# First tile of a fused attention and expert kernel: weight pieces, copies and zeros moved

## The chip, the cores and the metric

The kernel runs on one core of a Trainium2 chip. The metric is device time in microseconds (us). Engines are called TensorE, VectorE, ScalarE, GpSimd and SyncE; in the profile's rows they are PE (PEld for its weight loads), DVE, ACT, POOL and SP.

## What is computed

Three layers run one after the other: attention that keeps the 32 largest scores of a row, a gated FFN behind an RMS norm, and a switch of 8 experts, each token going to one of them.

```python
# q, k, v: (2, 8, 576, 64)
scores = scale * q @ k.T
kth = np.partition(scores, -32, axis=-1)[..., -32:-31]
scores = np.where(scores >= kth, scores, -1e9)
attn = softmax(scores); x = attn @ v          # -> (1152, 512)

xn = x / rms(x) * rms_g
x = (silu(xn @ w_gate) * (xn @ w_val)) @ w_out # d_ff 1536

e = argmax(x @ r_gate); p = softmax prob of e  # 8 experts
y = relu(x @ w1[e]) @ w2[e]; out = p * y       # capacity 288 rows an expert
```

## The kernel before

Tokens are cut into 9 tiles of 128 (`NT`). A group `g` is one pair of heads of one tile: 4 groups a tile (`HP`), 36 in all (`NG`). All engines walk the same list of slots `n` (0 to `SLOTS` - 1), and each has its own instruction order in a slot, written out by hand; they meet in semaphores only.

The attention is a pipeline over the slots. VectorE in slot n finds the 32 largest of each score row of group n (`vec.max` and `vec.match_replace`, L1160 to L1181, on rows of 576, two heads of 128 rows each). In slot n + 1 GpSimd makes the clip bias and the negative row maximum from that (`nbias`, L1335 and L1339). ScalarE marks what lies below the threshold (`marks`, L919), GpSimd takes the marks off the scores (the clip, L1348), ScalarE takes the exponentials (`probs`, L929) and copies the next group's scores out of PSUM (`score_rows`). TensorE makes those scores (`scores`, L452), turns the probabilities (`turn_probs`, L463) and multiplies them with the values (`values`, L479) at the slot's end. `out_columns` copies that product to `oT`; it comes a slot later, behind the marks. The product shares a bank of PSUM with the scores, so `scores(n + 1)` waits for it (L446).

The FFN of tile t lies in the same slots. `due(n, at, k)` tells whether step k of some tile falls in slot n at the place ALPHA, BETA or GAMMA (start, middle, end); tile t counts from slot `FIRST` + 4t, and `FIRST` is 6. So for tile 0: step XA (-4) is slot 4, end. There the attention columns of three head pairs are turned back (`turn_back_columns`), copied (`raw_rows`), normalized on GpSimd (`norm_first`, L1305 to L1310) and turned again (`turn_first_rows`); ScalarE then scales them by the gain into `x_hi` (`columns`). Step XB (-3) is the start of slot 5: the last pair's columns are turned (L555), copied (`raw_last_pair`), normalized (`norm_last`), turned (L557) and scaled; `squares` (L893) sums the squares for the RMS, which GpSimd finishes (`rms`), and VectorE makes the low parts `x_lo` (`low_part`, L1109). The gate blocks are `G` (slots 5, 6, 7), the value blocks `V` (slots 6, 7, 7), each of 12 matmuls (L496, L497, L500); the tanh (L798), the SiLU product on VectorE (L1101) and the multiply on GpSimd (L1293) follow. Then the output product (L509), the router and the dispatch of the tile's rows by an indirect DMA.

TensorE multiplies in `float32r` with operands split in a high and a low part. The FFN's weights are split on the chip, in 12 pieces of 128 x 1024 (`split_piece`): pieces 0, 1 are the first column block of `w_gate`, 2, 3 that of `w_val`, 4, 5 and 6, 7 the second blocks, 8, 9 and 10, 11 the third. ScalarE rounds a piece to its high part in two copies (`split_weights`), and GpSimd subtracts that from the piece (L1285). Both happen at the place that `SPLITS` names for the piece. On GpSimd the piece stands in `dense`, behind the slot's clips and ahead of the next slot's bias. Block i of tile 0 waits for the low parts it needs (L489).

SyncE issues the loads in a fixed order: keys, queries, values of batch 0, keys of batch 1, the gain, `w_gate`, `w_val`, the router; then 18 stores of zeros to the dispatch buffer and 9 to the output (L342 to L346), from `zrow`, the first 520 columns of `hid`. ScalarE waits for these stores in `squares(0)`, since it writes `hid` there. Then `w_out`, the next queries and the values of batch 1. `drow` is the row buffer in which tiles 0 to 7 put their FFN output before the dispatch.

At the end the experts run one after the other from their dispatched rows (L707, L721).

Of the kernel before, what the change touches and what calls it, by code (L numbers as in the profile page):

```python
# [47 lines left out]
LAST = 16  # L48
SPLITS = ((2, ALPHA), (2, GAMMA), (3, BETA), (3, GAMMA), (4, ALPHA), (4, GAMMA),
          (5, BETA), (5, GAMMA), (6, ALPHA), (6, BETA), (6, GAMMA), (7, ALPHA))  # L50


def build(nc, q, k, v, w_gate, w_val, w_out, rms_g, r_gate, w1, w2, out, capacity):
# [31 lines left out]
    with ctx:  # L85
# [52 lines left out]

        zrow = hid[:, 0:ROW]

# [40 lines left out]
        def gate_of(e, j):  # L181
# [15 lines left out]

            "k_turned k_acted k_veced k1_copied w_hi_set w_lo_set "

# [65 lines left out]

        def pieces(n, at):

            m = SPLITS.index((n, at)) if (n, at) in SPLITS else None
            return () if m is None else (m,)

# [27 lines left out]
        def _(sp):  # L298
# [44 lines left out]
            for i in range(SPOTS // P):  # L343
                sp.dma_start(disp[i * P:(i + 1) * P, :], zrow).then_inc(s["disp_zero"], 16)
            for i in range(NT):
# [55 lines left out]
        def _(pe):  # L401
# [82 lines left out]
            def ffn_block(t, parts, i, bank):  # L484


                if t == 0:

                    m = 4 * i + (2 if bank is blk[1] else 4)  # L489
                    pe.wait_ge(s["w_lo_set"], m)  # L490
                w_hi, w_lo = [w[:, :, i * 512:(i + 1) * 512] for w in parts]
                pe.wait_ge(s["x_hi_set"], CD * t + CD - 1)
                for c in range(CD):
                    if c == CD - 1:
                        pe.wait_ge(s["x_hi_set"], CD * (t + 1))
                    mm(bank, x_hi[:, c * P:(c + 1) * P], w_hi[:, c, :], start=(c == 0), stop=False)  # L496
                    mm(bank, x_hi[:, c * P:(c + 1) * P], w_lo[:, c, :], start=False, stop=False)  # L497
                pe.wait_ge(s["t_free"], use["xn", t] + 1)
                for c in range(CD):
                    last = mm(bank, x_lo[:, c * P:(c + 1) * P], w_hi[:, c, :], start=False, stop=(c == CD - 1))  # L500
                last.then_inc(s["blk_full"], 1)
# [119 lines left out]
            for n in range(SLOTS):  # L621
# [21 lines left out]
                else:  # L643
# [26 lines left out]
                    dense(n, GAMMA)  # L670
                    turn_first_rows(n)
                if probs:
                    if g == 0:
                        pe.wait_ge(s["v_in0"], 16 * 2 * KC)
                        pe.wait_ge(s["v_padded"], 2 * B)
                    if g == MIX * HP:
                        pe.wait_ge(s["v_in1"], 16 * 2 * KC)
                    values(g)

            stay_awake(AWAKE[1])  # L680
# [97 lines left out]
        def _(act):  # L778
# [49 lines left out]
            def dense(n, at):  # L828

                for m in pieces(n, at):  # L830
                    split_weights(m)
                for i in range(FB):
                    t = due(n, at, TANH[i])
                    if t is not None:
                        half_tanh(t, i)
                    t = due(n, at, V[i])
                    if t is not None:
                        value_block(t, i)
                t = due(n, at, LOGITS)
                if t is not None:  # L840
                    act.wait_ge(s["t_full"], use["lg", t] + 1)

                    if t > 0:
                        act.wait_ge(s["lexp_set"], t)
                    copy(lg[:], tb[:, 0:E]).then_inc(s["t_free"], 1)
                for i in range(FB):
                    t = due(n, at, HID[i])
                    if t is not None:
                        act.wait_ge(s["t_full"], use[f"h{i}", t] + 1)
                        copy(hid[:, i * 512:(i + 1) * 512], tb).then_inc(s["t_free"], 1)  # L850
                t = due(n, at, LEXP)
                if t is not None:

                    act.wait_ge(s["lneg_set"], t + 1)
                    nc.scalar.activation(lexp[:], lg[:], ACT.Exp, bias=rt[:, 1:2],
                                         accum_out=rt[:, 2:3]).then_inc(s["lexp_set"], 1)

            def out_rows(n):
                t = due(n, BETA, X2)
                if t is not None:  # L860
                    act.wait_ge(s["out_full"], t + 1)

                    if 0 < t < NT - 1:
                        act.wait_ge(s["dispatched"], t * 16)
                    copy(row_of(t)[:, 0:DM], blk[0]).then_inc(s["out_copied"], 1)
# [21 lines left out]
            def squares(t):  # L887
                act.wait_ge(s["normed"], 2 * t + 2)
                if t == 0:

                    act.wait_ge(s["disp_zero"], 16 * (SPOTS // P))
                    act.wait_ge(s["out_zero"], 16 * NT)
                nc.scalar.activation(sqr, xrow[:], ACT.Square,  # L893
# [59 lines left out]
            for n in range(SLOTS):  # L953
# [3 lines left out]
                if t is not None:  # L957
                    if 0 <= g - 1 < NG:
                        out_columns(g - 1)
                    if here:  # L960
                        marks(g, 0)
                    raw_last_pair(t)
                    if here:
                        marks(g, 1)
                    dense(n, ALPHA)
                    out_rows(n)
                    columns(t, (HP - 1,))
                    squares(t)
                    if here:
# [14 lines left out]
                    dense(n, GAMMA)  # L984
                else:
                    if here:
                        marks(g, 0)
                        marks(g, 1)
                    if 0 <= g - 1 < NG:
                        out_columns(g - 1)  # L990
                    if here:
# [26 lines left out]
                    dense(n, GAMMA)  # L1018
                    if t is not None:
                        columns(t, range(HP - 1))  # L1020

# [56 lines left out]
        def _(dve):  # L1078
# [34 lines left out]
            def beside(n, at):  # L1113

                for i in range(FB):
                    t = due(n, at, SILU[i])
# [112 lines left out]
        def _(pool):  # L1229
# [12 lines left out]
            gp.memset(nones[:], -1.0)  # L1242
            gp.memset(zrow, 0.0).then_inc(s["z_set"], 1)
            gp.iota(rt[:, 10:11].bitcast(I32), pattern=[[0, 1]], base=0, channel_multiplier=1).then_inc(s["pchain"], 1)
# [5 lines left out]
            gp.memset(zrow[:, DM + 1:DM + 2].bitcast(I32), NOTOK)  # L1250
            gp.memset(q_space[:, DM:ROW], 0.0)
            gp.memset(drow[:, DM:ROW], 0.0).then_inc(s["z_set"], 1)

# [8 lines left out]
            def dense(n, at):  # L1262
# [6 lines left out]
                if t is not None:  # L1269
# [10 lines left out]
                    gp.tensor_scalar(token[:], token[:], float(P), None, ALU.add)  # L1280
                for m in pieces(n, at):

# [44 lines left out]
            for n in range(SLOTS):  # L1327
                g = n - 1
                if 0 <= g < NG:
                    pool.wait_ge(s["th_set"], 2 * g + 2)  # L1330
# [6 lines left out]
                    if g > 1:  # L1337
                        pool.wait_ge(s["masked"], 2 * g - 2)
                    gp.tensor_scalar(nbias[:, 2 * (g % 2):2 * (g % 2) + 2].rearrange("p (a w) -> p a w", w=1), two[:, :, 0, 0:1], -1.0, None,  # L1339
                                     ALU.mult).then_inc(s["bias_set"], 1)  # L1340
                t = due(n, ALPHA, XB)
                if t is not None:
                    norm_last(t)
# [58 lines left out]
```

## Time and profile before

| | us |
|---|---|
| median of 3 runs (lowest, highest) | 686.82 (686.48, 688.23) |
| the profiled execution, its own time | 686.69 |
| its span, first to last instruction | 684.9 |
| TensorE busy | 614.4 (90%) |
| VectorE busy | 412.4 (60%) |
| ScalarE busy | 326.4 (48%) |
| GpSimd busy | 262.7 (38%) |

The mean granted TensorE clock is 0.962 of full speed. A row of a timeline gives start, duration, engine, line, operation, tiles and count, and in brackets how long the engine was idle before and what released it. A row of the chain gives start, duration and what the chain went through. Busy time of TensorE is modelled and says that work was there, not how fast it went.

### The profile page before, as it was taken

The page shows a single profiled execution, that of the slowest core. Times are in us where ns is not written, and L with a number is a line of the kernel's source. Part 1 is how long each engine was busy: PE and PEld are TensorE (multiplying, and loading weights), DVE is VectorE, ACT ScalarE, POOL GpSimd, SP SyncE. Part 2 cuts the span into 40 slices and gives each one's busy share as a digit, 9 for nine tenths or more (in the row PEclk, how much of TensorE's full clock was granted, in tenths as well). Part 3 has the DMA queues.
Part 4 walks back from the last instruction along what each step waited for, and adds up shares of the span by engine and source line. Part 5 has one row for each costly group of instructions (what it writes and reads, how often), then busy time and mean ns, then how long its engine had stood idle before and what let it go on. Part 6 is the DMA issues. An engine that isn't in the chain of part 4 may idle for free.

```text
span 684.9 us, 11003 instructions
## 1 busy us (share of the span) xinstructions
PE 614.4 (90%) x3882; PEld 475.4 (69%) x3882; DVE 412.4 (60%) x911; ACT 326.4 (48%) x713; POOL 262.7 (38%) x363
## 2 busy tenths in 40 slices
PE   5464578999999999999999999999988999999994
PEld 3343455576676675775775766756648999999994
DVE  4998488789799799699798897921100101111110
ACT  3576566675675675766757766743210111111010
POOL 1356586445355454544455454551210011111101
PEclk9775799999999999999999999999999999999998
DMA  9999100000000000010000000000448676678401
GB/s 187 347 380 343 37 17 0 1 16 17 1 15 17 2 21 13 1 32 1 17 17 0 1 17 1 1 17 0 177 124 313 221 272 225 229 260 276 160 7 37
DMA packets 53070, 65.45 MB, mean 96 GB/s; under 512 B 32218, under 2 KB 32218, under 8 KB 53020
## 3 DMA queue, kind: packets, MB, share of 16 engines
q1 hardware_dynamic: 51276, 60.05, 27.6%
q0 software_dynamic: 1744, 4.76, 1.9%
q8 instruction: 28, 0.46, 0.3%
q14 instruction: 22, 0.18, 0.1%
HBM read 52.89 MB, written 12.30 MB: 95 GB/s over the span
## 4 chain that ended last, share of the span: by engine, by line
PE 74%; ACT 9%; POOL 8%; issue 5%; DVE 3%; DMA 1%; SPq 0%; POOLq 0%; ACTq 0%; DVEq 0%
PE ps L707 11%; PE ps L509 11%; PE ps L721 11%; PE ps L496 7%; PE ps L500 7%; PE ps L497 7%; PE ps L479 4%; PE ps L452 4%; PE ps L463 4%; POOL w_parts L1285 3%; PE ps L437 3%; POOL s_ring L1348 2%; ACT pt L780 2%; ACT z_pair L919 2%; POOL hid L1293 1%
## 5 line engine op out<-in xcount | busy, mean ns | idle before, releaser
L1348 POOL TENSOR_TENSOR s_ring<-s_ring,z_pair 128x576 f32<-128x576 f32 x72 | 101.0, 1424 | 47.0 <-ACT z_pair L919 47.0
L1177 DVE MATCH_REPLACE8 w_top<-m,w_top 128x576 f32<-128x576 f32 x144 | 105.8, 742 | 0.0
L1173 DVE MAX8 m<-w_top 128x8 f32<-128x576 f32 x144 | 101.6, 747 | 0.0
L509 PE MATMUL ps<-wo_space,hid 128*128 128x512 f32 x216 | 100.1, 597 | 0.4 <-issue 0.4
L496 PE MATMUL ps<-w_parts,x_hi 128*128 128x512 f32 x216 | 90.1, 417 | 0.0
L497 PE MATMUL ps<-w_parts,x_hi 128*128 128x512 f32 x216 | 85.4, 395 | 0.0
L707 PE MATMUL ps<-arena,w_loads 128*128 128x168 f32 x512 | 76.0, 310 | 0.6 <-ACT arena L780 0.6
L721 PE MATMUL ps<-arena,w_loads 128*128 128x168 f32 x512 | 75.8, 307 | 0.6 <-issue 0.6
L707 PEld LDWEIGHTS ps<-arena,w_loads 128*128 128x128 f32 x512 | 75.0, 193 | 0.8 <-ACT arena L780 0.8
L1363 POOL DMA_INDIRECT out_rows<-arena,s_ring x16 | 15.1, 941 | 156.3 <-DVE arena L1200 153.8
L721 PEld LDWEIGHTS ps<-arena,w_loads 128*128 128x128 f32 x512 | 73.2, 190 | 0.9 <-issue 0.9
L919 ACT ACTIVATE z_pair<-s_ring,nbias 128x576 f32<-128x576 f32 x72 | 52.8, 777 | 32.4 <-POOL nbias L1335 32.4
L1160 DVE MAX8 m<-s_ring 128x8 f32<-128x576 f32 x72 | 52.4, 750 | 22.9 <-ACT s_ring L780 22.9
L929 ACT ACTIVATE s_ring<-s_ring,nbias 128x576 f32<-128x576 f32 x72 | 55.7, 774 | 20.1 <-POOL s_ring L1348 20.0
L452 PE MATMUL ps<-arena,q_cols 64*128 64x288 f32 (+1 forms) x320 | 49.2, 458 | 15.7 <-ACT oT L780 13.5
L509 PEld LDWEIGHTS ps<-wo_space,hid 128*128 128x128 f32 x216 | 37.7, 190 | 35.7 <-issue 35.7
L463 PE MATMUL ps<-ident,s_ring 128*128 128x128 f32 x288 | 47.4, 290 | 16.6 <-ACT s_ring L929 8.2
L500 PE MATMUL ps<-w_parts,x_lo 128*128 128x512 f32 x216 | 59.2, 396 | 0.0
L463 PEld LDWEIGHTS ps<-ident,s_ring 128*128 128x128 f32 x288 | 35.0, 148 | 31.8 <-ACT s_ring L929 14.8
L479 PE MATMUL ps<-pt,arena 128*64 128x128 f32 (+1 forms) x800 | 49.7, 274 | 7.8 <-ACT pt L780 7.8
L780 ACT ACTIVATE pt<-ps 128x512 f32<-128x512 f32 (+1 forms) x108 | 49.0, 491 | 10.5 <-PE ps L463 10.5
L1166 DVE MATCH_REPLACE8 w_top<-m,s_ring 128x576 f32<-128x576 f32 x72 | 53.2, 742 | 0.0
(125 smaller groups left out, 859.9 us busy)
## 6 DMA issues: line engine op xcount, KB each, us to landing
w_loads<-in_moe_w SPq DMA_DIRECT2D x16, 2048.0 KB, 9.0
dispatched_rows<-hid SPq DMA_DIRECT2D x18, 260.0 KB, 6.4
w_loads<-in_moe_w_gate SPq DMA_DIRECT2D x1, 3072.0 KB, 11.6
w_loads<-in_moe_w_val SPq DMA_DIRECT2D x1, 3072.0 KB, 19.1
wo_space<-in_moe_w_out SPq DMA_DIRECT2D x1, 3072.0 KB, 13.2
arena<-dispatched_rows SPq DMA_DIRECT2D x8, 341.2 KB
out_rows<-hid SPq DMA_DIRECT2D x9, 256.0 KB, 4.5
q_space<-in_q SPq DMA_DIRECT2D x8, 256.0 KB, 3.0
```

What stands on the lines that cost most here:

```text
L452: last = mm(ps[r0:r1, 2 * a + half, 0:HS], q_cols[a * D:(a + 1) * D, hp, r0:r1], kT[b][a * D:(a + 1) * D, hp, half * HS:(half + 1) * HS], ...
L463: last = tr(pt_ps[:, j * P:(j + 1) * P], s_ring[:, g % SR, a, a * KL + j * P:a * KL + (j + 1) * P], ident[:])
L479: last = mm(oT_ps[a * D:(a + 1) * D, r0:r1], vs[b][:, j, 2 * hp + a, :], pt[:, at + r0:at + r1], start=(j == 0), stop=(j == KC - 1))
L496: mm(bank, x_hi[:, c * P:(c + 1) * P], w_hi[:, c, :], start=(c == 0), stop=False)
L497: mm(bank, x_hi[:, c * P:(c + 1) * P], w_lo[:, c, :], start=False, stop=False)
L500: last = mm(bank, x_lo[:, c * P:(c + 1) * P], w_hi[:, c, :], start=False, stop=(c == CD - 1))
L509: last = mm(blk[0], hid[:, c * P:(c + 1) * P], wo_s[:, c, :], start=(c == 0), stop=(c == CF - 1))
L707: last = mm(ps[:, 2 + n % 2, (f % 2) * MAIN:(f % 2 + 1) * MAIN], w1_s[par][:, c, f * P:(f + 1) * P], xT[par][:, c, :], start=(c == 0), sto ...
L721: last = mm(ps[:, 4 + n, (d % 2) * MAIN:(d % 2 + 1) * MAIN], w2_s[par][:, f, d * P:(d + 1) * P], hT[:, f, :], start=(f == 0), stop=(f == C ...
L1173: vec.max(m8[:, 2 * (n % 2) + a, i, :], w_top[:, a, :]).then_inc(s["top_step"], 1)
L1177: vec.match_replace(w_top[:, a, :], m8[:, 2 * (n % 2) + a, i, :], w_top[:, a, :], NEG).then_inc(s["top_step"], 1)
L1348: gp.tensor_tensor(row, row, z_pair[:, a, :], ALU.subtract).then_inc(s["lowered"], 1)
```

## The change

- `SPLITS` becomes two tables and a third: ScalarE makes the high parts by `HIGH` (pieces 0 and 1 at the end of slot 1, 2 and 3 at the end of slot 2, 4 and 5 at the end of slot 3, 6 to 11 in slots 5 to 7), GpSimd the low parts of pieces 0 to 7 by `LOW` (pairs in slots 2, 3, 5 and 6; none in slot 4), VectorE those of pieces 8 to 11 by `LOW_VECTOR` (slots 6 and 7, in `beside`).
- ScalarE copies the attention columns ahead of the marks in all slots. The scaling of the first three pairs goes from the end of the XA slot to the start of the next, ahead of the marks too, as does the copy of the last pair. For tile 0 alone the last pair's scaling and the squares go ahead of the marks as well.
- GpSimd's `norm_last(0)` goes ahead of the slot's clip bias, for tile 0 alone.
- TensorE's `turn_first_rows` goes behind `values`, for all tiles.
- The zeros are stored from `drow`; ScalarE waits for the stores ahead of tile 0's output row.

```diff
-SPLITS = ((2, ALPHA), (2, GAMMA), (3, BETA), (3, GAMMA), (4, ALPHA), (4, GAMMA),
-          (5, BETA), (5, GAMMA), (6, ALPHA), (6, BETA), (6, GAMMA), (7, ALPHA))
+HIGH = ((1, GAMMA), (1, GAMMA), (2, GAMMA), (2, GAMMA), (3, GAMMA), (3, GAMMA),
+        (5, BETA), (5, GAMMA), (6, ALPHA), (6, GAMMA), (7, ALPHA), (7, BETA))
+LOW = ((2, ALPHA), (2, ALPHA), (3, ALPHA), (3, ALPHA), (5, BETA), (5, BETA), (6, BETA), (6, BETA))
+LOW_VECTOR = ((6, BETA), (6, GAMMA), (7, ALPHA), (7, BETA))
...
-        zrow = hid[:, 0:ROW]
+        zrow = drow
...
# TensorE, ffn_block of tile 0
-                    pe.wait_ge(s["w_lo_set"], m)
+                    pe.wait_ge(s["w_lo_set"], min(m, len(LOW)))
+                    if m > len(LOW):
+                        pe.wait_ge(s["w_low_veced"], m - len(LOW))
...
# TensorE, slot
                     dense(n, GAMMA)
-                    turn_first_rows(n)
...
                     values(g)
+                turn_first_rows(n)
...
# ScalarE, out_rows
+                    if t == 0:
+                        act.wait_ge(s["disp_zero"], 16 * (SPOTS // P))
+                        act.wait_ge(s["out_zero"], 16 * NT)
...
# ScalarE, XB slot
                         out_columns(g - 1)
+                    columns(t, range(HP - 1))
+                    raw_last_pair(t)
+                    if t == 0:
+                        columns(t, (HP - 1,))
+                        squares(t)
                     if here:
                         marks(g, 0)
-                    raw_last_pair(t)
-                    if here:
                         marks(g, 1)
                     dense(n, ALPHA)
                     out_rows(n)
-                    columns(t, (HP - 1,))
-                    squares(t)
+                    if t > 0:
+                        columns(t, (HP - 1,))
+                        squares(t)
...
# ScalarE, other slots
+                    if 0 <= g - 1 < NG:
+                        out_columns(g - 1)
                     if here:
                         marks(g, 0)
                         marks(g, 1)
-                    if 0 <= g - 1 < NG:
-                        out_columns(g - 1)
...
                     dense(n, GAMMA)
-                    if t is not None:
-                        columns(t, range(HP - 1))
...
# VectorE, beside
+                for m in pieces(LOW_VECTOR, n, at):
+                    raw, hi, lo, half, cols = split_piece(m + len(LOW))
+                    dve.wait_ge(s["w_hi_set"], 2 * (m + len(LOW)) + 2)
+                    vec.tensor_tensor(lo[:, half[0]:half[1] + 1, cols], raw[:, half[0]:half[1] + 1, cols],
+                                      hi[:, half[0]:half[1] + 1, cols], ALU.subtract).then_inc(s["w_low_veced"], 1)
...
# GpSimd, slot
             for n in range(SLOTS):
                 g = n - 1
+                t = due(n, ALPHA, XB)
+                if t == 0:
+                    norm_last(t)
...
-                t = due(n, ALPHA, XB)
-                if t is not None:
+                if t is not None and t > 0:
                     norm_last(t)
```

## Rows read from the trace of the kernel before

**Rows 1.** Page, part 1: busy us, share of the span, instructions of each engine.

```profile
PE 614.4 (90%) x3882; PEld 475.4 (69%) x3882; DVE 412.4 (60%) x911; ACT 326.4 (48%) x713; POOL 262.7 (38%) x363
```

**Rows 2.** Windows: busy us of PE, PEld, DVE, ACT, POOL; then clock, DMA share.

```profile
60.00:78.00 18.00, 7.97 (x45) 5.40 (x43) 9.85 (x20) 8.50 (x22) 9.39 (x10) 0.55 0.68 183
...
307.63:355.83 48.20, 47.03 (x290) 32.89 (x288) 43.02 (x97) 31.90 (x71) 24.14 (x36) 1.00 0.04 12
```

**Rows 3.** Chain of waits, 0 to 135 us: start, duration, what.

```profile
41.33 2.35 POOL w_parts L1285
...
43.76 0.21 POOL nbias L1335
...
54.34 2.35 POOL w_parts L1285
...
56.77 0.22 POOL nbias L1335
...
67.27 2.35 POOL w_parts L1285
...
100.43 2.39 POOL w_parts L1285
...
102.91 0.23 POOL nbias L1335
...
114.81 1.27 POOL hid L1293
...
116.16 0.23 POOL nbias L1335
```

**Rows 4.** Line 1285 (durations in ns, min/median/max), and the timeline of ScalarE's slot 4.

```profile
L1285 POOL TENSOR_TENSOR w_parts<-w_loads,w_parts x12: 2348/2364/2416, 35.6 to 107.4; 128x1024 fp32r<-128x1024 f32 x12
...
57.02 1.44 ACT L919 ACTIVATE z_pair<-s_ring,nbias 128x576 f32<-128x576 f32 x2 [3.39 <-POOL nbias L1335]
...
60.10 1.13 ACT L780 ACTIVATE w_parts<-w_loads 128x512 fp32r<-128x512 f32 x2
```

**Rows 5.** Timeline of VectorE, 50 to 95 us.

```profile
50.16 1.40 DVE L1160 MAX8 m<-s_ring 128x8 f32<-128x576 f32 x2
...
61.80 0.76 DVE L1160 MAX8 m<-s_ring 128x8 f32<-128x576 f32 x1 [1.91 <-ACT s_ring L780]
...
78.39 1.13 DVE L1109 SCALAR_TENSOR_TENSOR x_lo<-ps,gain,x_hi 128x128 fp32r<-128x128 f32 x4 [6.22 <-ACT x_hi L884]
...
86.53 0.69 DVE L1101 SCALAR_TENSOR_TENSOR hid<-hid,ps 128x512 f32<-128x512 f32 x1 [3.25 <-ACT hid L798]
...
93.41 1.41 DVE L1181 MAX8 m<-w_top 128x8 f32<-128x576 f32 x2
```

**Rows 6.** DMA issues: a row of SyncE's timeline, then KB and us to landing.

```profile
19.76 0.51 SPq L338 DMA_DIRECT2D w_loads<-in_moe_w_gate  x1
...
w_loads<-in_moe_w_gate SPq DMA_DIRECT2D x1, 3072.0 KB, 11.6
w_loads<-in_moe_w_val SPq DMA_DIRECT2D x1, 3072.0 KB, 19.1
```

**Rows 7.** Timeline of tile 0's chain in slot 5.

```profile
73.51 2.40 PE L479 MATMUL ps<-pt,arena 128*64 128x128 f32 x20
...
76.82 0.27 ACT L780 ACTIVATE xrow<-ps 128x128 f32<-128x128 f32 x1
...
77.53 2.80 POOL L1348 TENSOR_TENSOR s_ring<-s_ring,z_pair 128x576 f32<-128x576 f32 x2
...
78.26 0.62 ACT L893 ACTIVATE hid<-xrow 128x512 f32<-128x512 f32 x1
```

**Rows 8.** Timeline of a middle tile, slot 26 (TensorE and ScalarE).

```profile
331.68 1.31 PE L479 MATMUL ps<-pt,arena 128*64 128x128 f32 x20
...
332.14 1.46 ACT L919 ACTIVATE z_pair<-s_ring,nbias 128x576 f32<-128x576 f32 x2
...
337.58 0.60 PE L463 MATMUL ps<-ident,s_ring 128*128 128x128 f32 x4
```

More of the change, by code:

```diff
@@ L196, in build @@
             "disp_zero out_zero id_set z_set pchain v_padded "
-            "k_turned k_acted k_veced k1_copied w_hi_set w_lo_set "
+            "k_turned k_acted k_veced k1_copied w_hi_set w_lo_set w_low_veced "
             "t_full t_free vchain "
@@ L264, in split_piece, with pieces @@
             return raw, hi, lo, (2 * (m % 2), 2 * (m % 2) + 1), slice(j // 2 * 512, (j // 2 + 1) * 512)
-        def pieces(n, at):
-            m = SPLITS.index((n, at)) if (n, at) in SPLITS else None
-            return () if m is None else (m,)
+        def pieces(table, n, at):
+            return [m for m, place in enumerate(table) if place == (n, at)]
         def next_tile(n):
@@ L343, in _ @@
             for i in range(SPOTS // P):
-                sp.dma_start(disp[i * P:(i + 1) * P, :], zrow).then_inc(s["disp_zero"], 16)
+                sp.dma_start(disp[i * P:(i + 1) * P, :], zrow[:]).then_inc(s["disp_zero"], 16)
             for i in range(NT):
@@ L828, in dense @@
             def dense(n, at):
-                for m in pieces(n, at):
+                for m in pieces(HIGH, n, at):
                     split_weights(m)
@@ L888, in squares @@
                 act.wait_ge(s["normed"], 2 * t + 2)
-                if t == 0:
-                    act.wait_ge(s["disp_zero"], 16 * (SPOTS // P))
-                    act.wait_ge(s["out_zero"], 16 * NT)
                 nc.scalar.activation(sqr, xrow[:], ACT.Square,
@@ L1242, in _ @@
             gp.memset(nones[:], -1.0)
-            gp.memset(zrow, 0.0).then_inc(s["z_set"], 1)
+            gp.memset(zrow[:], 0.0).then_inc(s["z_set"], 1)
             gp.iota(rt[:, 10:11].bitcast(I32), pattern=[[0, 1]], base=0, channel_multiplier=1).then_inc(s["pchain"], 1)
@@ L1250, in _ @@
             gp.memset(zrow[:, DM + 1:DM + 2].bitcast(I32), NOTOK)
-            gp.memset(q_space[:, DM:ROW], 0.0)
-            gp.memset(drow[:, DM:ROW], 0.0).then_inc(s["z_set"], 1)
+            gp.memset(q_space[:, DM:ROW], 0.0).then_inc(s["z_set"], 1)
             steps = [0]
@@ L1280, in dense @@
                     gp.tensor_scalar(token[:], token[:], float(P), None, ALU.add)
-                for m in pieces(n, at):
+                for m in pieces(LOW, n, at):
                     raw, hi, lo, half, cols = split_piece(m)
```

## The prediction

> **What bounds the kernel now.** I read the windows by stretch first. A tile in the middle (four slots) lasts 48.20 us and TensorE is busy for 47.03 of it at the full granted clock, so no order of the other engines can give more than 1.2 us per tile there [rows 2]. The stretch 60 to 78 us is the other extreme: TensorE busy for 7.97 of 18 us, at a mean granted clock of 0.55 [rows 2]. Page part 1 (TensorE 90%) averages the two [rows 1]. So the change is worth what it saves before tile 0's FFN joins the rhythm.
>
> The chain of waits says what holds that stretch [rows 3]. GpSimd runs the low weight pieces (L1285, 2.35 us each), and each slot's clip bias (L1335) stands behind them in its queue: 41.33 + 2.35 leads to the bias at 43.76, 54.34 + 2.35 to 56.77, 67.27 + 2.35 to the normalization, 100.43 + 2.39 to 102.91. The first wait of another kind is at 114.81: the multiply of the third value block, then the bias of slot 8 at 116.16. In the middle of the kernel that pair recurs every 48.2 us, so the rhythm starts there. The question is how much earlier that bias comes; whatever it gains reaches the end unless the new order costs TensorE time per tile.
>
> VectorE has a rhythm too, the top-32 search, 9.64 us a slot without idle time up to slot 4's start at 50.16; slot 5's first maximum waits 1.91 us for its score rows [rows 5]. No slot of the start can be shorter than that.
>
> **Part by part.** Times "new" are added up by me in queue order from durations of the rows; those "before" are in the rows.
>
> *High pieces a slot ahead (ScalarE).* A piece is two copies, 1.13 us, 1.04 to the next start [rows 4]. Pieces 0 and 1 now stand at the end of slot 1, where ScalarE is free from 29.4. Their weights were issued at 19.76 and landed 11.6 later, at 31.4 [rows 6]. So ScalarE ends at 33.5, and slot 2's marks start 2.2 us late. VectorE doesn't see it: slot 3's score rows are ready at about 38.7 and it wants them at 40.52, two slots of 9.64 ahead of 59.8. Pieces 2 and 3 come at 41.8, after theirs have landed (issued right behind, at 19.76 + 0.51, and 19.1 later: 39.4 [rows 6]), and end at 43.9: slot 3's marks start at 44.1 (before: right behind the bias of 43.76, so nothing won yet). GpSimd does low pieces 0 and 1 from 37.4 to 42.2, before slot 3's search result needs it.
>
> *Slots 3 and 4.* Clips end at 47.8, low pieces 2 and 3 at 52.5 (before 56.69), the bias comes at 52.6. ScalarE has high pieces 4 and 5 until 53.2; the attention columns wait for TensorE's product of slot 3 (2.40 us at the half clock, the form of the row at 73.51 [rows 7]), end at 53.7, and the marks start there, against 57.02 [rows 4]: 3.3 earlier. Copying the columns in front of the marks lets TensorE score beside the clips, and the piece of 60.10 [rows 4] is gone: another 1.1. The slot's probabilities end at 58.1, the raw rows at 61.65: 4.4 earlier than before. Slot 5's search starts at 59.8 instead of 61.80.
>
> *Tile 0's chain.* No low piece stands ahead of the normalization now (2.35, and 1.2 of waiting for its high part). The reciprocals run beside the transposes, and the first rows are scaled at 62.5. Moving the transpose of the first rows behind the product adds 2.40 there, but the product had to be done before the last pair anyway. So: product ends 63.6, transpose 64.5, three column copies 65.4, last pair copied 65.65 (before 76.82 + 0.27), scaled 66.1, last column 66.85, squares 67.55 (before 78.26 + 0.7 [rows 7]): 11.4 earlier. The marks, now behind all this, start at 67.6 and the clips end at 71.2, against 77.53 + 2.80 = 80.33 [rows 7]: 9.1 earlier. GpSimd's scaling of the last pair now stands ahead of the bias in its queue; ScalarE would not be free for the marks sooner, so that is free.
>
> *Slots 5 to 7.* RMS follows at 72.8; VectorE's low parts wait for its own search, 59.8 + 9.64, and end at 70.6; the first gate block ends at 71.6 at full clock. Two high pieces and the turned rows put the first tanh at 75.9 and its SiLU at 76.6, against 86.53 [rows 5]: 9.9 earlier. GpSimd does low pieces 4 and 5 from 72.8 to 77.5, its clips to 81.5, the multiply, and 6 and 7 from 83.9 to 88.7: slot 7's bias at 88.7, against 102.91 [rows 3], 14.2 earlier.
>
> *The last four low pieces on VectorE.* No row shows this operation there. 128x512 with two inputs took 0.69 and 128x128 0.28 (four in 1.13) [rows 5]; extended by that slope, 128x1024 is 1.2, 1.13 from start to start. The nearest row above is GpSimd's 2.35; the bound below is 0.69. From the SiLU at 76.6 VectorE works without a pause: the rest of its search used 86.53 to 94.82 [rows 5], so slot 6's threshold is at 86.05 with one piece in it. Slot 7 is 9.64, one SiLU of 0.6 and three pieces, 3.4; the last piece ends ahead of the closing maxima (1.3), at 98.4. TensorE's third value block (2.85) waits for that one and ends at 101.3, where it alone would be done by 99. Copy 0.70, multiply 1.3: the bias of slot 8 at 103.5 against 116.16 [rows 3]: 12.6 earlier. VectorE is what is late next, GpSimd no longer.
>
> *Zeros from the row buffer.* The same bytes from another tile in the same place of SP's queue; the GpSimd fill keeps its size. The two waits moved to tile 0's output row are met some 50 us before. Nothing.
>
> *The later tiles.* For t > 0 the squares and last column stay behind the marks; ScalarE has the marks 0.4 to 0.9 later in those slots. VectorE idles afterwards until a SiLU and absorbs it; TensorE's operands are still there in time. Columns ahead of marks delay the marks where the product ends late: 331.68 + 1.31 against marks at 332.14 [rows 8], 1.1 us. TensorE asks for the masked rows at 337.58 [rows 8], and they would be ready at 336.4. Slack remains: zero, bounds -0.1 to +0.3 per tile, -1 to +2.4 in all.
>
> **Sum.** 12.6, less 1.2 for about 25 hand-offs between engines on the new path, each of which I took 0.05 shorter than the 0.1 that the chain shows: 11.4. The span goes from 684.9 to 673.5; with the 1.8 us around it (686.69 - 684.9) 675.3, and as the median 686.82 stands 0.1 above the profiled execution, **675.4 us**.
>
> **A rule weighed against the change.** In the trace before, every large VectorE instruction reads one tile of SBUF and at most one of PSUM, and GpSimd's 2.35 us pieces ran the same length whatever VectorE did (2348 to 2416 ns) [rows 4]. The Trainium skill's page SBUF — State Buffer, section Who interferes with whom, says that a VectorE instruction with two SBUF inputs and a GpSimd instruction that reads SBUF exclude each other, and the later one waits for the whole of the earlier. No run here has shown such a pair; the new subtractions on VectorE are the first.
>
> **Rivals.**
> 1. *The new VectorE pieces and GpSimd's operations get in each other's way.* Piece 8 falls (83.6) beside GpSimd's pieces 6 and 7, piece 9 and 10 beside clips and a multiply. Were each of the first three to wait half to all of a GpSimd operation of 2.35, 1.42 or 1.3 us, VectorE, the late engine, loses 2.5 to 5: 678 to 680. For it: the new form. Against: they need not overlap. By the page's rule this is what would happen, in part at least.
> 2. *TensorE's clock.* The products of the start ran at half the clock: 2.40 for what later took 1.31 [rows 7, 8]. In the new order TensorE has about 2 us of gaps between 64.8 and 68.8. If it is granted 0.5 there and in the first gate block, that takes 2.9 and the scores 1.1 longer, 3.5 through to the SiLU: 678.9. Against: it works from 59 to 64.8 nearly without pause.
> 3. *More than forecast*: VectorE's pieces cost 0.7 or the hand-offs nothing: 673 to 674.
> 4. *Slower.* ScalarE's column copy ahead of the marks, in every slot of every tile: 1.1 and 1.0 us later in two slots of four [rows 8]. It decides from the point where it is more than the 1.2 us left before TensorE asks for the masked rows; if the following value block's copy and the score rows add to it and all of it shows, 2.1 x 8 = 16.8: 692.
> 5. *No change*: the early slots are held by weight transfers. Against it: both landed by 39.4 [rows 6].
>
> **Chances.** Forecast (673 to 677.3) 0.57; rivals 1 and 2 together, 677.3 to 681.5, 0.25; rival 3, below 673, 0.07; a smaller gain, to 684.7, 0.04; no change 0.03; rival 4 0.04. The range 671.5 to 681.5 leaves out some 0.13. A measurement tells about 0.3%, 2 us, from nothing: faster 0.93, same 0.03, slower 0.04.
>
> **What would show it.** Right: slot 8's bias near 104.7; slot 5's search starts at 59.8; GpSimd's normalization before 63; the tile period still 48.2; the VectorE subtraction near 1.2. Wrong: high pieces 0 and 1 wait past 33; subtractions of 2 us, or GpSimd clips longer than 1.43; the first gate block at half clock; a tile period of 48.5 or more.

## The result and the profile after

The changed kernel takes 677.77 us (median of 4 runs, 677.38 to 679.16), the kernel before beside it 687.53 us (4 runs, 686.48 to 688.27). The ratio is 0.9863, 95% interval 0.9841 to 0.9885: 9.4 us faster by the ratio (the two medians differ by 9.8). The profiled execution has a span of 676.1 us, against 684.9, so 8.8 us less, at a mean granted TensorE clock of 0.964. The forecast was 675.4 us and 11.4 us less.

Page, part 1, of the changed kernel (busy us, share, instructions), to be held against [rows 1]:

```profile
PE 614.7 (91%) x3882; PEld 474.3 (70%) x3882; DVE 418.3 (62%) x915; ACT 326.9 (48%) x713; POOL 256.7 (38%) x358
```

The work is the same to a few us: VectorE has 4 instructions and 6 us more, GpSimd 5 fewer and 6 us less. The windows say where the 8.8 us came from; their columns are those of [rows 2].

```profile
60.00:78.00 18.00, 13.25 (x86) 9.69 (x85) 14.48 (x33) 12.60 (x30) 11.40 (x15) 0.90 0.61 167
97.50:106.94 9.44, 7.05 (x41) 5.09 (x40) 9.44 (x19) 2.60 (x6) 1.28 (x1) 0.82 0.00 0
298.40:346.60 48.20, 47.03 (x290) 32.80 (x286) 43.07 (x97) 31.95 (x71) 24.24 (x36) 1.00 0.05 12
```

The hole of 60 to 78 us is filled: TensorE works 13.25 of 18 us there (7.97 before), at 0.90 of the clock (0.55). The third window was laid 48.20 us long, as that of the kernel before, and holds the same 47.03 us of TensorE; the period itself is read further below, from the multiply that recurs. The second window is the place where the forecast lost its time: between 97.5 us and slot 8's bias VectorE never rests (9.44 of 9.44), TensorE does for a quarter of the time, and its granted clock is 0.82.

The chain of waits of the changed kernel, from the first gate block to slot 8's bias (start, duration, what it went through); it answers to [rows 3]:

```profile
70.37 1.21 PE ps L504 x4
...
83.12 3.04 issue
...
89.61 1.13 DVE w_parts L1124
...
98.75 1.14 DVE w_parts L1124
99.89 0.25 issue
...
103.06 1.68 PE ps L504 x4
...
105.59 1.27 POOL hid L1303
106.94 0.23 POOL nbias L1348
```

In the kernel before the chain went through GpSimd's low pieces; none is left in it. It runs through VectorE's search and the four new subtractions (L1124), and comes to slot 8's bias at 106.94, 9.22 us earlier than 116.16. Of the forecast's 12.6 that leaves 3.4 missing. Two things are to be seen: the 3.04 us of "issue" at 83.12, in which VectorE did nothing that the chain can name, and the last subtraction's end at 99.89, for which TensorE waited.

The timelines name both. VectorE of the changed kernel (start, duration, engine, line, operation, tiles, count, idle before and its releaser), against [rows 5]:

```profile
75.99 0.69 DVE L1106 SCALAR_TENSOR_TENSOR hid<-hid,ps 128x512 f32<-128x512 f32 x1 [3.03 <-ACT hid L802]
...
82.87 3.37 DVE L1124 TENSOR_TENSOR w_parts<-w_loads,w_parts 128x1024 fp32r<-128x1024 f32 x1
...
89.53 1.21 DVE L1124 TENSOR_TENSOR w_parts<-w_loads,w_parts 128x1024 fp32r<-128x1024 f32 x1
...
94.76 1.21 DVE L1124 TENSOR_TENSOR w_parts<-w_loads,w_parts 128x1024 fp32r<-128x1024 f32 x1
...
98.67 1.21 DVE L1124 TENSOR_TENSOR w_parts<-w_loads,w_parts 128x1024 fp32r<-128x1024 f32 x1
```

GpSimd of the changed kernel, with the same columns:

```profile
60.91 0.84 POOL L1307 TENSOR_TENSOR xrow<-xrow,rden 128x384 f32<-128x384 f32 x1 [1.68 <-ACT xrow L784]
...
71.53 4.68 POOL L1295 TENSOR_TENSOR w_parts<-w_loads,w_parts 128x1024 fp32r<-128x1024 f32 x2
...
82.78 5.69 POOL L1295 TENSOR_TENSOR w_parts<-w_loads,w_parts 128x1024 fp32r<-128x1024 f32 x2
88.55 0.22 POOL L1348 TENSOR_SCALAR nbias<-m 128x2 f32<-128x2 f32 x1
...
89.67 3.73 POOL L1360 TENSOR_TENSOR s_ring<-s_ring,z_pair 128x576 f32<-128x576 f32 x2 [0.60 <-ACT z_pair L922]
94.69 2.42 POOL L1303 TENSOR_TENSOR hid<-xrow,hid 128x512 f32<-128x512 f32 x1 [1.29 <-ACT xrow L812]
```

Lay the two side by side. The subtraction takes 1.21 us three times and 3.37 once. That one begins at 82.87, just behind GpSimd's first piece of a pair (82.78). This piece would be done at 82.78 + 2.35 = 85.13, and 85.13 + 1.13 = 86.26 is the subtraction's end (82.87 + 3.37 = 86.24): it waited for the whole of GpSimd's instruction and then ran at its own speed. GpSimd's second piece then waited for it: 5.69 for the pair, where the pair at 71.53, with no subtraction beside it, took 4.68. The other way round, piece 9 at 89.53 came first and the clip waited (3.73 for the 2.80 of [rows 7]), and the multiply beside piece 10 took 2.42 for the 1.27 that the one at 105.59 in the chain took. By the Trainium skill, page SBUF — State Buffer, section Who interferes with whom, a VectorE instruction with two SBUF inputs and a GpSimd instruction that reads SBUF exclude each other, the later one waiting for all of the earlier; by that rule, the trace agrees. But where two recorded starts lie within 0.1 us, the rows don't tell which of the two will wait: the multiply's row begins 0.07 us ahead of piece 10's (94.69 and 94.76), and it is the one that was stretched. In keep_awake (rows below) the same two begin 0.08 apart, again the multiply first, and there the subtraction waited.

TensorE of the changed kernel at the third value block:

```profile
100.14 0.47 PE L500 MATMUL ps<-w_parts,x_hi 128*128 128x512 f32 x1 [2.39 <-DVE w_parts L1124]
100.44 0.40 PE L501 MATMUL ps<-w_parts,x_hi 128*128 128x512 f32 x1
...
101.57 0.63 PE L501 MATMUL ps<-w_parts,x_hi 128*128 128x512 f32 x1
```

It idled 2.39 us for the last subtraction. The block begins with matmuls of 0.40 us, and from 101.1 they take 0.63: the clock fell from the 2.4 to the 1.2 GHz level inside it. The twelve took 4.6 us; at the full clock they take 2.96 (in no_inputs below 98.94 to 101.90).

### The profile page after: what moved, and what is told of

It reads as the page before. It is cut to its first block, busy times and chain, and to the rows that moved or that the text cites. A ratio compares the mean times of both kernels' runs of the same rounds, so it can differ in the third digit from the quotient of the medians.

```text
span 676.1 us, 11004 instructions
## 1 busy us (share of the span) xinstructions
PE 614.7 (91%) x3882; PEld 474.3 (70%) x3882; DVE 418.3 (62%) x915; ACT 326.9 (48%) x713; POOL 256.7 (38%) x358
## 4 chain that ended last, share of the span: by engine, by line
PE 73%; DVE 11%; ACT 6%; issue 5%; POOL 4%; DMA 1%; SPq 0%; POOLq 0%; DVEq 0%; ACTq 0%
PE ps L711 11%; PE ps L725 11%; PE ps L513 11%; PE ps L500 7%; PE ps L504 7%; PE ps L501 7%; PE ps L481 4%; PE ps L454 4%; PE ps L465 4%; DVE w_top L1188 3%; DVE m L1184 3%; PE ps L439 3%; POOL s_ring L1360 2%; DVE w_top L1177 2%; POOL hid L1303 2%
## 5 line engine op out<-in xcount | busy, mean ns | idle before, releaser
L481 PEld LDWEIGHTS ps<-pt,arena 128*64 128x64 f32 x800 | 42.1, 143 | 19.7 <-issue 10.4
L500 PEld LDWEIGHTS ps<-w_parts,x_hi 128*128 128x128 f32 x216 | 40.7, 189 | 17.1 <-issue 9.6
```

The source lines that it names most:

```text
L481: last = mm(oT_ps[a * D:(a + 1) * D, r0:r1], vs[b][:, j, 2 * hp + a, :], pt[:, at + r0:at + r1], start=(j == 0), stop=(j == KC - 1))
```

## The experiments

All kernels beside the one before, with the number that decides, the start of slot 8's bias. The last column is the span less that start. The intervals are of the ratio to the kernel before, which ran on the same chip.

| kernel | slot 8's bias | span | median | ratio (95%) | the rest |
|---|---|---|---|---|---|
| before | 116.16 | 684.9 | 687.53 | 1 | 568.7 |
| changed | 106.94 | 676.1 | 677.77 | 0.9863 (0.9841 to 0.9885) | 569.2 |
| changed once more (after_again) | 107.71 | 678.7 | 679.04 | 0.9875 (0.9853 to 0.9897) | 571.0 |
| low_gpsimd | 108.21 | 675.8 | 677.92 | 0.9896 (0.9877 to 0.9915) | 567.6 |
| no_inputs | 104.19 | 673.4 | 675.33 | 0.9844 (0.9817 to 0.9872) | 569.2 |
| keep_awake | 105.97 | 677.0 | 676.85 | 0.9873 (0.9849 to 0.9896) | 571.0 |
| vector_early | 106.28 | 674.1 | 674.06 | 0.9844 (0.9817 to 0.9871) | 567.8 |
| tables_only | 109.72 | 679.5 | 679.99 | 0.9892 (0.9873 to 0.9911) | 569.8 |
| order_only | 114.71 | 681.5 | 685.07 | 0.9971 (0.9959 to 0.9983) | 566.8 |
| both_early | 104.72 | 674.0 | 674.75 | 0.9821 (0.9791 to 0.9851) | 569.3 |
| both_again | 105.21 | 672.0 | 675.86 | 0.9844 (0.9814 to 0.9875) | 566.8 |
| apart | 102.55 | 670.5 | 672.68 | 0.9813 (0.9784 to 0.9841) | 568.0 |

The rest is 566.8 to 571.0 with no order in it: what the start gains reaches the end, but one execution's span is worth 2 us either way. So the traces are compared up to slot 8's bias, and the times by their medians.

**Is the subtraction long because GpSimd is beside it?** no_inputs keeps every wait and place and takes the reading away; it leaves the low parts of the third blocks out of the result.

```diff
-                    vec.tensor_tensor(lo[...], raw[...], hi[...], ALU.subtract).then_inc(s["w_low_veced"], 1)
+                    vec.memset(lo[...].bitcast(F32), 0.0).then_inc(s["w_low_veced"], 1)
```

> The changed kernel with the four subtractions on VectorE replaced by fills of zeros of the same size and waits: they read nothing from SBUF, so the low parts of the third blocks are left out of the result. My theory (a VectorE instruction with two SBUF inputs and GpSimd's instructions exclude each other): the piece that took 3.37 takes 1.1, GpSimd's clip of 2.3 goes back to 1.4 and its multiply of 2.42 to 1.28, the third value block starts by 98 and runs at full clock, slot 8's bias comes near 103.3 instead of 106.9: about 674. Rival (the long instructions come from something else, such as the wait for the high part): 677.8 and the same long instructions of GpSimd.

VectorE and GpSimd of no_inputs (timeline), and TensorE at the third value block:

```profile
84.11 0.91 DVE L1124 MEMSET w_parts<- 128x1024 f32 x1 [0.16 <-issue]
```

```profile
84.25 4.74 POOL L1294 TENSOR_TENSOR w_parts<-w_loads,w_parts 128x1024 fp32r<-128x1024 f32 x2
...
90.18 2.82 POOL L1359 TENSOR_TENSOR s_ring<-s_ring,z_pair 128x576 f32<-128x576 f32 x2 [0.60 <-ACT z_pair L922]
94.28 1.30 POOL L1302 TENSOR_TENSOR hid<-xrow,hid 128x512 f32<-128x512 f32 x1 [1.28 <-ACT xrow L812]
```

```profile
98.94 0.47 PE L500 MATMUL ps<-w_parts,x_hi 128*128 128x512 f32 x1 [1.60 <-DVE w_parts L1124]
...
101.90 1.31 PE L481 MATMUL ps<-pt,arena 128*64 128x128 f32 x20
```

The four fills overlap GpSimd's operations at the same places and take 0.91 us each; all of GpSimd's stretched operations are back at 4.74, 2.82 and 1.30. A VectorE instruction that reads nothing doesn't hold GpSimd and isn't held; the one that reads two tiles is. The bias comes at 104.19, 2.75 earlier, although its first SiLU ran 1.0 later than in the changed kernel (76.99 against 75.99), so the overlaps and what followed from them are worth more than the 2.75. Two other things are in that number. The third value block ran at the full clock here, 2.96 us for 4.6, and the fill is by itself 0.3 us shorter than a subtraction, 4 x 0.3 in all; the share of the overlaps alone can't be told apart here.

**Was it right to take the pieces off GpSimd?** low_gpsimd leaves pieces 8 to 11 there.

```diff
-LOW = (..., (6, BETA), (6, BETA))
-LOW_VECTOR = ((6, BETA), (6, GAMMA), (7, ALPHA), (7, BETA))
+LOW = (..., (6, BETA), (6, BETA), (6, BETA), (6, GAMMA), (7, ALPHA), (7, BETA))
+LOW_VECTOR = ()
```

> The changed kernel with the low parts of pieces 8 to 11 on GpSimd, at the same places, instead of on VectorE. My theory (the placing on VectorE is a gain, though the two engines get in each other's way there): GpSimd has two more pieces of 2.35 ahead of slot 7's bias (88.5 becomes about 92.3) and two more in slot 7, the third value block starts near 103 instead of 100.1, slot 8's bias comes 3 us later: about 681, and no GpSimd clip longer than 1.43. Rival (the interference eats what the move brings): 677 to 678, as the changed kernel.

GpSimd of low_gpsimd, then TensorE's wait for the third value block:

```profile
82.53 9.42 POOL L1296 TENSOR_TENSOR w_parts<-w_loads,w_parts 128x1024 fp32r<-128x1024 f32 x4
```

```profile
102.95 0.47 PE L501 MATMUL ps<-w_parts,x_hi 128*128 128x512 f32 x1 [1.29 <-issue]
```

Slot 7's bias and the block's start fell where they were expected, 92.03 (82.53 + 9.42, and 0.08) and 102.95. But the block ran at the full clock throughout (the third gate block, behind an idle time of 3.94, at the half one), so the bias came only 1.3 later than in the changed kernel (0.5 later than in after_again). The time came out as the rival had it (677 to 678), not as I had expected (681): the ratios 0.9896 and 0.9863, or 0.9875 for after_again, have intervals that overlap, and their distance is 1.4 to 2.3 us where I had expected 3. Moving the four pieces to VectorE did bring the block's start 2.8 us forward (102.95 to 100.14), overlaps and all; 1.6 of that went in the half clock that the block met in the changed kernel and not here.

**What does the half clock in the third value block cost?** keep_awake gives TensorE something to do while it waits.

```diff
+                    if m > len(LOW) and bank is blk[0]:
+                        pe.wait_ge(s["wo_in"], 16)
+                        for c in range(2):
+                            mm(bank[:, 0:384], ident[:], wo_s[:, c, 0:384], start=True, stop=True)
```

> The changed kernel with two unused products of 384 columns in TensorE's wait ahead of the third value block (into the bank that the block then overwrites). Theory (the half clock in that block comes of TensorE's 2.4 us of idling ahead of it): the block takes 2.95 instead of 4.6 us, slot 8's bias comes 1.65 earlier: about 676.1. Rival (the clock falls for another reason, or the idle time does not matter to it): 677.8.

TensorE of keep_awake; the first row is the added products:

```profile
97.18 1.46 PE L496 MATMUL ps<-wo_space,ident 128*128 128x384 f32 x4
100.62 0.50 PE L504 MATMUL ps<-w_parts,x_hi 128*128 128x512 f32 x1 [1.99 <-DVE w_parts L1128]
```

GpSimd's multiply and VectorE's piece 10 in keep_awake, to be held against 94.69 and 94.76 of the changed kernel:

```profile
94.28 1.29 POOL L1307 TENSOR_TENSOR hid<-xrow,hid 128x512 f32<-128x512 f32 x1 [1.29 <-ACT xrow L816]
```

```profile
94.36 2.30 DVE L1128 TENSOR_TENSOR w_parts<-w_loads,w_parts 128x1024 fp32r<-128x1024 f32 x1
```

The block starts 0.5 later (its subtractions took 2.82, 1.21, 2.30, 1.21) and yet slot 8's bias comes 1.0 earlier, at 105.97: the block takes 3.07 us, 100.62 to 103.69. That is 1.5 us for the clock, of the 1.65 expected. The ratios, 0.9873 and 0.9863, don't show it.

**Do earlier pieces miss the overlaps?** vector_early moves the high pieces 6 to 11 and VectorE's four one place ahead.

```diff
-        (5, BETA), (5, GAMMA), (6, ALPHA), (6, GAMMA), (7, ALPHA), (7, BETA))
+        (4, GAMMA), (4, GAMMA), (5, BETA), (5, GAMMA), (6, ALPHA), (6, GAMMA))
-LOW_VECTOR = ((6, BETA), (6, GAMMA), (7, ALPHA), (7, BETA))
+LOW_VECTOR = ((5, GAMMA), (6, BETA), (6, GAMMA), (7, ALPHA))
```

> The changed kernel with pieces 8 to 11 one place earlier on VectorE (slot 5's end, 6's middle, 6's end, 7's start) and high pieces 6 to 11 on ScalarE earlier (two at slot 4's end, where it idles for 1.9 us, then one each at the former places of 6 to 9). Theory (VectorE is what is late, by the last piece, and it idles 3.0 us ahead of the first SiLU): the first piece lies in that idle time, the last is done before TensorE asks, the third value block starts at about 97.8 instead of 100.1 and at full clock, slot 8's bias comes about 4 us earlier: 674. Rival (TensorE, ScalarE or GpSimd stand behind VectorE by less than 1 us): 677.

TensorE of vector_early at the second value block:

```profile
91.61 0.47 PE L500 MATMUL ps<-w_parts,x_hi 128*128 128x512 f32 x1 [2.14 <-issue]
```

The third block waited for nothing now, but began at 101.02 where I had expected 97.8, for the subtractions still met GpSimd (1.97, 1.22, 1.28, 1.89; its pairs took 5.67 twice), and the second value block waited 2.14 for GpSimd's piece 7 and half of it ran at the half clock. The bias came at 106.28, 0.7 us earlier than in the changed kernel, not 4. The time that I had forecast, 674, came all the same (674.06); it isn't a hit of the theory, whose gain at the bias didn't come, and the interval (0.9817 to 0.9871) overlaps that of the changed kernel. The wait had moved from VectorE back to GpSimd.

**Which half of the change gives the gain?** tables_only has the new tables in the old order, order_only the new order with the old twelve places.

```diff
# order_only
+HIGH = ((2, ALPHA), (2, GAMMA), (3, BETA), (3, GAMMA), (4, ALPHA), (4, GAMMA),
+        (5, BETA), (5, GAMMA), (6, ALPHA), (6, BETA), (6, GAMMA), (7, ALPHA))
+LOW = HIGH
+LOW_VECTOR = ()
```

```diff
# tables_only: TensorE, ScalarE and GpSimd as before the change
-                turn_first_rows(n)
...
-                    columns(t, range(HP - 1))
-                    raw_last_pair(t)
...
-                if t == 0:
-                    norm_last(t)
```

> The kernel before with the tables of the weight pieces alone (high parts ahead, low parts by LOW and LOW_VECTOR); columns, squares, the first rows' transpose and the last pair's scaling in their old places. My theory (tile 0 was held by GpSimd's low pieces ahead of its normalization and its biases): nearly all of the gain of 9.2 us at slot 8's bias is here, the bias comes at 107 to 108.5, time 678 to 679. Rival (the order carries half): bias at 111, 682.

> The changed kernel with the old places of all 12 pieces, high part on ScalarE and low part on GpSimd: the new order alone. My theory: GpSimd's piece at the end of slot 4 still stands ahead of the normalization (first rows scaled at about 71, before 71.79, changed 60.91), slot 8's bias comes 1 to 3 us earlier than before's 116.16: 684 to 686. Rival (the order carries half): bias at 111 or earlier, 682 or less.

TensorE's wait for the third value block in tables_only, and the scaling of the first rows on ScalarE in order_only:

```profile
102.03 0.77 PE L500 MATMUL ps<-w_parts,x_hi 128*128 128x512 f32 x1 [3.49 <-DVE w_parts L1122]
```

```profile
72.87 0.88 ACT L891 ACTIVATE x_hi<-ps,gain 128x128 fp32r<-128x128 f32 x3 [5.24 <-PE ps L439]
```

The tables alone give 7.4 us (1.08% of 687.8), the order alone 2.0 (0.29%, 12 runs, interval clear of 1). The sum is that of the whole change, 9.4 (8.6 by after_again, on the same chip as these two). tables_only's bias came 1.2 later than the end of my range: it waited 3.49 us, and then the whole block ran at the half clock. Its time, 679.99, is a us above the expected 678 to 679. order_only shows why the order is worth so little alone: with the low pieces still ahead of GpSimd's normalization, ScalarE's scaling by the gain comes at 72.87, where the changed kernel has it at 63.51, and ScalarE stood 5.24 us.

**Does the remedy for both waits beat the change?** both_early is vector_early with one of GpSimd's pieces drawn ahead to slot 4, behind the normalization of tile 0.

```diff
-LOW = (..., (5, BETA), (5, BETA), (6, BETA), (6, BETA))
+LOW = (..., (4, 3), (5, BETA), (5, BETA), (6, BETA))
...
                     norm_first(t)
+                low_pieces(n, 3)
```

> As the kernel with pieces 8 to 11 earlier, and GpSimd's low pieces earlier too: piece 4 right behind the scaling of the first rows, where GpSimd idled for 2.9 us, 5 and 6 where 4 and 5 were, 7 alone in slot 6. Theory (with VectorE relieved, the second value block waited 2.1 us for GpSimd's piece 7, with the half clock behind it): that block starts at about 88 instead of 91.6, no wait ahead of the third one, slot 8's bias near 102.3 against 106.94 in the changed kernel: 673. Rival (piece 4 delays the last pair's scaling, or the engines block each other more): bias at 105, 676.

GpSimd of both_early, then VectorE's piece 9:

```profile
87.69 0.22 POOL L1351 TENSOR_SCALAR nbias<-m 128x2 f32<-128x2 f32 x1 [2.50 <-DVE m L1192]
...
103.37 1.27 POOL L1306 TENSOR_TENSOR hid<-xrow,hid 128x512 f32<-128x512 f32 x1 [9.51 <-DVE hid L1106]
```

```profile
83.27 3.00 DVE L1124 TENSOR_TENSOR w_parts<-w_loads,w_parts 128x1024 fp32r<-128x1024 f32 x1
```

TensorE is nearly clear: second value block at 87.08 without a wait, third at 96.81 behind 1.22 us, both at the full clock. The bias missed the expected 102.3 by 2.4 all the same, and came where the rival had it (105), and the releasers say for whom it waited: GpSimd stood 2.50 us for VectorE's maxima and 9.51 for its third SiLU. VectorE's subtractions took 2.53, 3.00, 1.76 and 1.21, 3.7 more than four times 1.21. VectorE itself was late, by the overlaps.

**The same pieces, kept apart.** apart gives piece 8 to GpSimd, into the 2.50 us in which it stood, and puts piece 9 where VectorE would find GpSimd between its clips and its multiply.

```diff
-LOW = (..., (4, 3), (5, BETA), (5, BETA), (6, BETA))
-LOW_VECTOR = ((5, GAMMA), (6, BETA), (6, GAMMA), (7, ALPHA))
+LOW = (..., (4, 3), (5, BETA), (5, BETA), (6, BETA), (6, BETA))
+LOW_VECTOR = ((6, ALPHA), (6, GAMMA), (7, ALPHA))
```

> As both_early, but the low part of piece 8 goes to GpSimd's pair of slot 6 (where GpSimd waited 2.50 us for VectorE's maxima), and VectorE does piece 9 in the middle of slot 6's search, about 80.3 us, between GpSimd's clips (end 80.25) and its multiply (81.5); pieces 10 and 11 stay. By exclusion only piece 10 can meet a GpSimd operation: the subtractions take 1.2 us each, at most one longer than 1.4, GpSimd's pair 4.7, slot 7's bias stays near 87.6, the SiLU of the third block comes 2.4 us earlier (102.62 to 100.2) and slot 8's bias at 102.3 instead of 104.72: 672.3 us. If the lost time in both_early is not the overlap but VectorE's plain amount of work, only one piece of 1.2 us is saved: bias at 103.5, 673.6 us. If TensorE's half clock falls in a block again, 1.5 to 2 us more than either.

> The kernel both_early once more, beside the run of apart: slot 8's bias at 104.2 to 105.2 and 674 to 676 us where the overlaps fall as before. Piece 9's subtraction beside GpSimd's piece between 2.3 and 3.4 us. Were the bias to move by more than 1 us between two executions of the same kernel, the difference to apart would have to be read from the medians alone.

VectorE's pieces 9 and 11 in apart, then GpSimd:

```profile
80.34 1.52 DVE L1124 TENSOR_TENSOR w_parts<-w_loads,w_parts 128x1024 fp32r<-128x1024 f32 x1
...
93.17 1.21 DVE L1124 TENSOR_TENSOR w_parts<-w_loads,w_parts 128x1024 fp32r<-128x1024 f32 x1
```

```profile
83.31 4.70 POOL L1277 TENSOR_TENSOR w_parts<-w_loads,w_parts 128x1024 fp32r<-128x1024 f32 x2
...
93.15 2.37 POOL L1306 TENSOR_TENSOR hid<-xrow,hid 128x512 f32<-128x512 f32 x1 [0.25 <-ACT xrow L812]
...
102.55 0.22 POOL L1351 TENSOR_SCALAR nbias<-m 128x2 f32<-128x2 f32 x1
```

Slot 8's bias comes at 102.55 (102.3 expected; 103.5 if only the amount of VectorE's work counted), and the median is 672.68 us (672.3 expected). In both_again the subtractions took 3.23, 2.97, 1.76 and 1.21, and the bias came at 105.21. In apart the three took 1.52, 1.21 and 1.21: the first met the end of GpSimd's clips (77.97 + 2.81 = 80.78), and the other two weren't held, but GpSimd's bias and multiply beside them were (1.11 and 2.37). The bias is 2.7 us earlier. One piece less on VectorE can be 1.1 to 1.2 of that; the other 1.5 hang on where the pieces lie. The forecast of 102.3 was made from the exclusion. apart's interval ends where the changed kernel's begins (0.9841 both), and it lies 0.005 below the first, 0.006 below after_again: it has the lowest ratio here, some 4 us ahead of the changed kernel. From both_early and both_again (0.9821 and 0.9844) its interval isn't clear.

**The changed kernel once more.**

> The changed kernel once more, on the same chip as the three others: the bar to hold them against. 0.986 of before, as in its first runs, and slot 8's bias near 106.9 (107.2 less or more by the start's variation of 0.3 us).

TensorE of after_again at the end of slot 5 and at the third value block:

```profile
75.46 2.40 PE L481 MATMUL ps<-pt,arena 128*64 128x128 f32 x20 [0.64 <-ACT pt L784]
...
100.90 0.47 PE L500 MATMUL ps<-w_parts,x_hi 128*128 128x512 f32 x1 [1.67 <-DVE w_parts L1124]
```

In this execution the overlaps were kinder (1.49, 1.47, 1.23, 1.22, though GpSimd's pair took 5.72), and the clock less so: it also fell at the end of the first gate block (70.1 us), and the product at 75.46 took 2.40 instead of 1.31. The bias came 0.8 later than in the first, more than the 0.3 that I had allowed. Within one kernel both effects shift from execution to execution, and trade places.

## Why the prediction was right in sign and 2.4 us short in time

The result, 677.77, lies in the range (671.5 to 681.5), but just above the likeliest case (673 to 677.3), in the band that belonged to rivals 1 and 2 together. Step by step:

- *What holds the start.* Right. The hole was GpSimd's queue, and without the pieces ahead of the normalization GpSimd has scaled the first rows by 60.91 + 0.84 = 61.75 (forecast 62.5). order_only and tables_only confirm it from both sides.
- *The hand-made schedule up to slot 7.* Right, 0.2 to 1.8 us pessimistic. ScalarE:

```profile
30.27 2.19 ACT L784 ACTIVATE w_parts<-w_loads 128x512 fp32r<-128x512 f32 x4 [1.11 <-DMA w_loads<-in_moe_w_gate]
...
52.61 1.43 ACT L922 ACTIVATE z_pair<-s_ring,nbias 128x576 f32<-128x576 f32 x2
...
65.73 0.62 ACT L896 ACTIVATE hid<-xrow 128x512 f32<-128x512 f32 x1
```

  High pieces 0 and 1 end at 32.5 (33.5; the weights landed a us earlier than in the trace before), slot 4's marks start at 52.61 (53.7), the squares end at 66.35 (67.55), slot 5's search starts at 59.56 (59.8), the SiLU at 75.99 (76.6), slot 7's bias at 88.55 (88.7). This last agreement is two errors that cancel: GpSimd began its pair 1.1 early and took 1.0 longer over it.
- *The allowance of 1.2 us for hand-offs.* Not needed up to there; every station came before its forecast, not behind it. It stood in for losses that came from elsewhere: of the 3.4 us missing at slot 8's bias it covered 1.2, and that the time came out only 2.4 us above the forecast is luck to that extent. (The recorded terms of that bias, 98.4 + 2.85 + 0.70 + 1.3, add up to 103.25; the 103.5 has 0.25 more that no row gives.)
- *The last four low pieces on VectorE.* **This is the step that failed.** "128x1024 is 1.2, 1.13 from start to start" holds for the instruction alone (1.21, and 1.13 in the chain), and the bounds 0.69 to 2.35 didn't hold the one that counted, 3.37. VectorE lost 2.2 us there. Two recorded signs of being wrong came true with it, a subtraction above 2 us and GpSimd clips above 1.43 (3.73 for two). As it had come 0.6 early, the last piece was done at 99.89 instead of 98.4: 1.5 us of the missing 3.4.
- *TensorE's third value block.* I gave it 2.85 us at the full clock, and looked for a half clock only at 64.8 to 68.8 us and in the first gate block (rival 2). In the first trace the clock held there (rows of 0.40 and 1.21 at 70.37) and fell here, behind the wait of 2.39 us: 4.6 us, 1.7 more. With 0.25 from the subtraction to the first matmul that makes 1.5 + 0.25 + 1.7 = 3.4. keep_awake shows the clock's part by itself. That the clock fell *because* of the wait isn't shown: with products in the wait it held, in one trace, but elsewhere it held behind longer waits (2.53 and 2.29 us, last section).
- *Rival 1.* Its mechanism is shown, by no_inputs and by the forecast of apart. Its time, 678 to 680, was worked out with three losses on VectorE; in the first trace GpSimd took two of the three, where it had slack; in keep_awake VectorE took two (2.82 and 2.30). Its chance was too low: the form of the instruction was the reason for it, and my "they need not overlap" had no row behind it. GpSimd's pair was forecast for 83.9 to 88.7 and piece 8 for 83.6, side by side, in the very same text.
- *Rival 4, and the later tiles.* The multiply of the third value block recurs once a tile. Three of its rows in the chain of the changed kernel:

```profile
298.30 1.28 POOL hid L1303
...
346.44 1.28 POOL hid L1303
...
394.57 1.28 POOL hid L1303
```

  The period is 48.14 and 48.13 us; before it was 48.20 (307.63, 355.83) and 48.18 (404.01). The multiply stands 9.22 us ahead at tile 0 and 9.44 six tiles later (394.57 against 404.01). So copying the columns ahead of the marks costs nothing that shows. Of these 9.4 us 0.6 are lost again, before the experts and not in them: their first product starts at 506.82 against 515.65, the last group at 656.95 against 665.78, 8.83 both times. That is within the 2 us by which the part behind slot 8 moves anyway.
- *Zeros from the row buffer: nothing.* I saw no wait for them, and tried no kernel that changes this alone. It stays unshown.

## What to carry to other kernels

When work is moved to another engine, its price isn't the duration it has alone: lay the new places over the timeline of the engine it may not run beside, and look for a hole there. A VectorE operation with two operands in SBUF beside GpSimd is such a pair; laying the pieces apart was worth some 1.5 us at the bias here, with one piece fewer on VectorE 2.7. And a TensorE wait can cost more than itself: the block behind it took 4.6 us here where it takes 2.96 at the full clock, so count it at both levels.

## What the runs showed of the hardware

- A VectorE subtraction of 128x1024 with both operands in SBUF takes 1.21 us alone and 3.37, 3.23, 3.17, 3.00, 2.97, 2.82 where its row starts behind that of a GpSimd piece that was still running; GpSimd's operation is stretched by 0.9 to 1.1 us where it comes second. Which one comes second can't be read from starts within 0.1 us. The fill of the same tile (0.91 us) neither waits nor makes wait. Even a bias of 128x2 on GpSimd took 1.07 to 1.11 instead of 0.22 beside such a subtraction (after_again, at 90.10; both_again, at 75.98; apart, at 88.10).
- A copy of the same kernel can lose the clock in one execution and keep it in the next: at the low-part matmuls of the first gate block the idle time ahead was 1.70 us in the changed kernel and 1.79 in after_again, and the first kept the 2.4 GHz level. At the third value block the clock held behind idle times of 1.22, 1.29 and 1.60 us, and of 1.99 behind the added products; it fell behind 1.67, 2.39 and 3.49, behind 3.94 at low_gpsimd's third gate block, and behind 2.14 at vector_early's second value block. But the length of the wait doesn't sort them: at the low-part matmuls of the first gate block the 2.4 GHz level held behind 2.04 (both_again), 2.29 (low_gpsimd) and 2.53 (keep_awake, the row below), all longer than the 1.67 behind which it fell. And in vector_early it was low at 76.83 (0.79 and 0.63 us a matmul), though no wait since 70.48 was longer than 1.31 us.

```profile
70.51 1.20 PE L508 MATMUL ps<-w_parts,x_lo 128*128 128x512 f32 x4 [2.53 <-DVE x_lo L1118]
```
